# Attention inside a three-stage kernel: the ninth transpose block moves to the PSUM bank of the output rows

## The chip, the cores and the metric

The kernel runs on one core of one Trainium2 chip. The metric is the device time of one execution in microseconds (us). Three runs of the kernel before took 985.68, 984.39 and 983.36 us; the median is 984.39 us.

## The reference

The input is attention over 4 batches of 8 heads, 576 positions, head size 64. Its output goes through a mixture of 8 experts (2304 rows of 512, hidden size 1024) and then through a dense layer with hidden size 2048. Only the first stage is touched by the change:

```
scores = q @ k.T / 8
keep only scores >= rowmax - tau, the others become -1e9
attn = exp(scores - rowmax) / (sum + 1e-9)
x = attn @ v                                  # (4*576, 8*64)
expert of a row = argmax(x @ w_gate + modality_bias)
```

## The kernel before, in words

The attention phase handles the heads in 16 pairs. The 576 query rows of a pair are cut into 5 tiles: four of 128 queries (for both heads of the pair), and a fifth that holds the last 64 queries of both heads together. This gives 80 steps; step n has the tile number n % 5 (0 to 4). The fifth tile (n % 5 = 4) has half the score columns of the others. A batch is 20 steps.

A step passes through these pieces of work, each on its own engine and each some loop turns later than the one before. In loop turn c the engines issue, in this fixed order:

- TensorE: `scores(c)` (lines 419 to 426), `pv(c-4)` (the V products, lines 494, 497, 509), `rows_out(c-5)` (a product that turns the outputs back into rows and forms the gate logits, lines 526 and 532), `turn(c-2)` (transposes of the probabilities, lines 448 for most tiles, 471 to 477 for tile 1), and once in a batch, at its turn number 7, `ranks` (lines 537 and 538).
- VectorE: `copy_scores(c)` twice (line 705: scores out of PSUM, with the row minimum), `invert`, `probs(c-1)` twice (line 718: mask, multiply, sum), `normalise(c-5)` for tiles 1, 3 and 4 (lines 746 or 750 and 752: rows out of PSUM), then small pieces of the routing (`choose`, `place`, `fill_rows` and others) in the 15 to 18 turns of a batch after the first batch is done.
- ScalarE: `exps(c)` first half (line 583), `copy_out(c-4)` (line 606: V products out of PSUM), `exps(c)` second half, `evacuate(c-2)` (lines 592 to 599: first the rest block of the transposes, then the main part), and in 16 turns `lead_high` (line 613).
- GpSimd: `find_limit(c)` (line 339), `add_eps`, and weight splitting or scatters in some turns.

Each engine works through its list in order, and a wait at one piece holds all that is behind it on that engine. Scores have one set of banks, so `scores(c)` waits until VectorE has copied the scores of turn c-1. `turn(c-2)` waits until ScalarE has evacuated the turn before it.

The eight PSUM banks: 0 to 3 hold scores, 4 and 5 the main part of the transposes (`turn_bank`). A full tile has nine blocks to transpose and eight fit in banks 4 and 5; the ninth (`rest_bank`) lies in bank 6, columns 0 to 127. The output of the V products (`ot_bank`) lies in the same bank 6, columns 128 to 255. Bank 7 holds the ranks (columns 0 to 47), one moved column (48) and the rows of `rows_out` (`row_bank`, columns 224 to 511). Tile 4 has only eight blocks and does not use `rest_bank`. Because ScalarE reads the V products out of bank 6, the first transpose into bank 6 has a wait of its own, `other_bank()`: step n waits until `copy_out(n-2)` is done. For tiles 0, 2 and 3 this wait stands ahead of the first transpose of the step, for tile 1 ahead of the last one.

```
def other_bank():
    if n >= 2:
        pe.wait_ge(ot_out, min(n - 1, NS - 3))
```

Of the kernel before, what the change touches and what calls it, by code (L numbers as in the profile page):

```python
# [21 lines left out]
P = 128  # L22
B, H, S, D = 4, 8, 576, 64
# [70 lines left out]
def attention_phase(nc, t, io):  # L94
# [107 lines left out]

    ahead_in_p = bterm[:, 0:TT + 1]
    a_bank, b_bank = psum[:, 0:2, 0:HALF], psum[:, 2:4, 0:HALF]
    turn_bank, rest_bank = psum[:, 4:6, :], psum[:, 6, 0:P]
    FAR = S

    def by_half(n):
# [194 lines left out]
    def tensor(pe):  # L403
# [24 lines left out]
        def turn(n):  # L428
            w, full = n % 3, n % TT < QT
            if n == 0:  # L430
                pe.wait_ge(consts, ALL_CONSTS)
            pe.wait_ge(prob_done, units(n) + 1)
            if n >= 1:
                pe.wait_ge(main_out, n)
            if n >= 1:
                pe.wait_ge(rest_out, n)
            blocks = QT if not full else 2 * QT

            def other_bank():

                if n >= 2:
                    pe.wait_ge(ot_out, min(n - 1, NS - 3))

            if by_half(n):
                def half_block(place, h, b):
                    rows = slice(h * D, h * D + D)
                    key = b * P if b < QT else (S + REM + (b - QT) * P if b < 2 * QT else QT * P)
                    return pe.transpose(place, prob[rows, w, key:key + P], ident[rows, rows])  # L448

                if full:  # L450
                    other_bank()
                    half_block(rest_bank[:, D:2 * D], 1, 0).then_inc(far_turned, 1)
                else:
                    half_block(turn_bank[:, 1, 0:D], 1, 0)
                half_block(turn_bank[:, 0, 0:D], 0, 0)
                for b in range(1, blocks):
                    if b == QT:
                        pe.wait_ge(prob_done, units(n + 1))
                    at = b - full
                    half_block(turn_bank[:, 1, at * D:at * D + D], 1, b)  # L460
                    half_block(turn_bank[:, 0, b * D:b * D + D], 0, b)
                at = blocks - full
                half_block(turn_bank[:, 1, at * D:at * D + D], 1, 2 * QT)
                if full:
                    pe.wait_ge(far_turned, halved(n))
                    half_block(rest_bank[:, 0:D], 0, 2 * QT).then_inc(turned, 1)
                else:
                    half_block(turn_bank[:, 0, QT * D:QT * D + D], 0, 2 * QT).then_inc(turned, 1)
                return
            for j in range(QT):  # L470
                pe.transpose(turn_bank[:, 0, j * P:(j + 1) * P], prob[:, w, j * P:(j + 1) * P], ident[:])
            pe.wait_ge(prob_done, units(n + 1))
            for j in range(QT):
                pe.transpose(turn_bank[:, 1, j * P:(j + 1) * P],
                             prob[:, w, S + REM + j * P:S + REM + (j + 1) * P], ident[:])
            other_bank()
            pe.transpose(rest_bank, prob[:, w, QT * P:QT * P + P], ident[:]).then_inc(turned, 1)

        def pv(n):
            p, tt = divmod(n, TT)  # L480
            u, w = p % 2, n % 2
            if tt == 0:
                pe.wait_ge(v_in[u], 16 * (p // 2 + 1))
            pe.wait_ge(main_out, n + 1)
            pe.wait_ge(rest_out, n + 2 if n < NS - 3 else n + 1)
            if n == NS - 3:
                pe.wait_ge(copied, units(NS - 1))
            elif 1 <= n < NS - 1:
                pe.wait_ge(ot_out, n)
            ot = ot_bank(n)  # L490
            if tt < QT:
                for j in range(QT):
                    for h in range(2):
                        pe.matmul(ot[h * D:(h + 1) * D, :], vsb[:, u, (h * QT + j) * D:(h * QT + j + 1) * D],  # L494
                                  turned_block(n, h * QT + j), start=(j == 0), stop=False)
                for h in range(2):
                    last = pe.matmul(ot[h * D:(h + 1) * D, :], vsb[:, u, VBD + h * D:VBD + (h + 1) * D],
                                     turned_block(n, 2 * QT), start=False, stop=True)
                last.then_inc(pv_done, 1)
            else:  # L500
                for j in range(QT + 1):
                    for h in range(2):
                        if j < QT:
                            v = vsb[:, u, VTURN + j * D:VTURN + (j + 1) * D] if h else vsb[:, u, j * D:(j + 1) * D]
                            pr = pt[:, w, h * FAR + j * D:h * FAR + (j + 1) * D]
                        else:
                            v = vsb[:, u, VREST + h * D:VREST + (h + 1) * D]
                            pr = pt[:, w, h * FAR + QT * D:h * FAR + (QT + 1) * D]
                        last = pe.matmul(ot[h * D:(h + 1) * D, 0:REM], v, pr, start=(j == 0), stop=(j == QT))
                last.then_inc(pv_done, 1)  # L510

        def rows_out(n):

            p, tt = divmod(n, TT)
            if n == 0:
                pe.wait_ge(wx_done, 4 * HP)
            pe.wait_ge(ot_out, n + 1)
            if n >= 1:
                pe.wait_ge(x_done, norms(n))
            b, k = divmod(n + 4 - ROUTE - RANK, PER)  # L520
            if k == 0 and b >= 0:
                pe.wait_ge(ranks_read, b + 1)
            c = (tt % 2) * 2 * HW
            for h in range(2):
                rows = slice(h * D, h * D + D)
                last = pe.matmul(row_bank[rows, c:c + 2 * HW], otsb[:, n % 2, rows],
                                 wx[:, p % HP].rearrange("p h c -> p (h c)"), start=True, stop=True)
            if tt == QT:
                pe.wait_ge(summed, norms(n + 1))
                for h in range(2):  # L530
                    rows = slice(h * D, h * D + D)
                    last = pe.matmul(moved[rows], t["shift"][:, rows], rsum[:, p % 2, 2 * QT:TPP], start=True, stop=True)
            last.then_inc(rows_done, 1)
# [7 lines left out]
        for c in range(NS):  # L541
            scores(c)
            if c >= 4:
                pv(c - 4)
            if c >= 5:
                rows_out(c - 5)
            if c >= 2:
                turn(c - 2)
            b, k = divmod(c - ROUTE, PER)
            if b >= 0 and k == RANK:  # L550
                ranks(b)
        turn_x, up_half, down = early["pe"](pe)
        pv(NS - 4)
        pe.wait_ge(copied, units(NS - 1))
# [104 lines left out]
    def vector(dve):  # L659
# [74 lines left out]
        def normalise(n):  # L734
            p, tt = divmod(n, TT)
            b, i = divmod(p, HP)
            if tt % 2 == 0 and tt < QT:
                return
            if i == 0 and tt == 1 and b >= 2:
                dve.wait_ge(scattered, 16 * TT * (b - 1))  # L740
            dve.wait_ge(rows_done, n + 1)
            cols = slice(i * 2 * HW, (i + 1) * 2 * HW)
            if tt < QT:
                settled()
                r = rinv[:, 2 * tt - 2:2 * tt + 2].rearrange("p (t h) -> p t h", h=2).unsqueeze(3)
                dve.tensor_tensor(x[:, b % 2, tt - 1:tt + 1, cols].rearrange("p t (h c) -> p t h c", h=2),
                                  row_bank.rearrange("p (t h c) -> p t h c", t=2, h=2),
                                  r.to_broadcast([P, 2, 2, HW]), ALU.mult).then_inc(x_done, 1)
            else:
                step(dve.reciprocal(rinv[0:REM, TPP:TPP + 1], moved[0:REM]))  # L750
                r = rinv[0:REM, 2 * QT:2 * TT].unsqueeze(2)
                dve.tensor_tensor(x[0:REM, b % 2, QT, cols].rearrange("p (h c) -> p h c", h=2),
                                  row_bank[0:REM, 0:2 * HW].rearrange("p (h c) -> p h c", h=2),
                                  r.to_broadcast([REM, 2, HW]), ALU.mult).then_inc(x_done, 1)
# [31 lines left out]
        def place(b, k):  # L786
# [2 lines left out]
            settled()  # L789
            if k == 0:  # L790
                dve.wait_ge(rank_done, b + 1)
                ranks = rank_bank.rearrange("p (t e) -> p t e", e=E)
                note(dve.tensor_tensor(lg[:], ranks[:, 0:TT], base8[:].unsqueeze(1).to_broadcast(wide), ALU.add))
                settled()
# [929 lines left out]
```

## Time and profile before

| | us |
|---|---|
| median of three runs | 984.39 |
| the profiled execution | 985.06 |
| its span, first to last instruction | 983.4 |
| TensorE busy | 919.6 (94%) |
| VectorE busy | 676.5 (69%) |
| ScalarE busy | 513.5 (52%) |
| GpSimd busy | 478.1 (49%) |
| mean granted TensorE clock | 0.994 |

The attention phase takes roughly the first third of the span; the experts and the dense layer take the rest. The busy shares are means over all phases, so they do not say what limits the attention phase.

### The profile page before, as it was taken

How to read it: one execution, taken by the hardware profiler on the slowest of the kernel's cores; microseconds unless marked ns; L12 is line 12 of the kernel's file. 1: busy time of each engine (PE TensorE's matmuls, PEld its weight loads, DVE VectorE, ACT ScalarE, POOL GpSimd, SP SyncE). 2: the span in 40 equal slices, each digit the busy share in tenths (PEclk: the TensorE clock that was granted, in tenths of full speed). 3: DMA queues.
4: the chain of work that ended last, by engine and by line, in shares of the span. 5: the costliest groups of instructions: out<-in, count | busy, mean ns of one | idle time of the engine just before them, and what ended most of it. 6: DMA issues, size and time to landing. Idle time of an engine off the chain costs nothing.

```text
span 983.4 us, 19418 instructions
## 1 busy us (share of the span) xinstructions
PE 919.6 (94%) x6976; PEld 773.0 (79%) x6977; DVE 676.5 (69%) x1227; ACT 513.5 (52%) x987; POOL 478.1 (49%) x560
## 2 busy tenths in 40 slices
PE   6888898889889999999999997999999999999997
PEld 4676676667667878888887896888988899889995
DVE  6887888788875641111125399888888888888793
ACT  5666666777665242222235455555455545555452
POOL 4222225465432275300000077786777786777784
PEclk9999999999999999999999999999999999999999
DMA  3122128223212457211125300100100100000000
GB/s 125 50 75 73 50 56 323 80 74 110 69 35 68 168 175 244 77 45 45 47 76 198 116 1 0 34 33 1 32 33 1 32 33 1 15 18 1 33 1 33
DMA packets 21937, 65.97 MB, mean 67 GB/s; under 512 B 3552, under 2 KB 3552, under 8 KB 21600
## 3 DMA queue, kind: packets, MB, share of 16 engines
q1 hardware_dynamic: 14512, 39.90, 12.0%
q0 software_dynamic: 4896, 20.00, 6.1%
q10 hardware_dynamic: 2448, 5.01, 1.7%
q8 instruction: 49, 0.80, 0.3%
q14 instruction: 32, 0.26, 0.1%
HBM read 46.63 MB, written 18.27 MB: 66 GB/s over the span
## 4 chain that ended last, share of the span: by engine, by line
PE 59%; DVE 5%; issue 3%; ACT 1%; ACTq 0%; POOL 0%; DVEq 0%; POOLq 0%
PE psum L1419 6%; PE psum L1421 6%; PE psum L1420 6%; PE psum L1411 6%; PE psum L1409 6%; PE psum L1410 6%; PE psum L1082 3%; PE psum L1084 3%; PE psum L1083 3%; PE psum L1109 3%; PE psum L1111 3%; PE psum L1110 3%; DVE rr L1531 2%; PE psum L1093 2%; PE psum L1068 1%
## 5 line engine op out<-in xcount | busy, mean ns | idle before, releaser
L1531 DVE RECIPROCAL rr<-rr 128x384 f32<-128x384 f32 x96 | 244.1, 2543 | 10.0 <-ACT rr L1479 10.0
L583 ACT ACTIVATE prob<-ssb,smin 128x576 f32<-128x576 f32 x144 | 111.6, 776 | 72.2 <-DVE ssb L705 72.2
L1357 POOL TENSOR_TENSOR uu<-uu,ex 128x384 f32<-128x384 f32 x96 | 97.3, 1014 | 100.6 <-ACT uu L1473 100.6
L705 DVE TENSOR_SCALAR_CACHE_REDUCE ssb<-psum,tauk 128x576 f32<-128x576 f32 x144 | 112.5, 815 | 46.7 <-PE psum L422 46.2
L1409 PE MATMUL psum<-x2T_hi,w_in_hi 128*128 128x384 f32 x384 | 130.8, 341 | 4.3 <-DVE gg L1537 2.7
L339 POOL TENSOR_TENSOR limit<-smin,margin 128x2 f32<-128x2 f32 (+1 forms) x80 | 58.1, 726 | 152.2 <-DVE ssb L705 151.7
L1411 PE MATMUL psum<-x2T_hi,w_in_lo 128*128 128x384 f32 x384 | 129.3, 337 | 0.0
L1410 PE MATMUL psum<-x2T_lo,w_in_hi 128*128 128x384 f32 x384 | 128.7, 335 | 0.0
L1163 DVE TENSOR_TENSOR hT_lo<-psum,hT_hi 128x512 fp32r<-128x512 f32 x38 | 26.3, 691 | 140.8 <-ACT hT_hi L1140 140.8
L1419 PE MATMUL psum<-w_hi,g_hi 128*128 128x512 f32 x288 | 114.0, 396 | 0.1
L1421 PE MATMUL psum<-w_hi,g_lo 128*128 128x512 f32 x288 | 113.8, 395 | 0.0
L1420 PE MATMUL psum<-w_lo,g_hi 128*128 128x512 f32 x288 | 113.7, 395 | 0.0
L1479 ACT ACTIVATE rr<-uu 128x384 f32<-128x384 f32 x96 | 50.5, 526 | 118.6 <-POOL uu L1357 118.6
L1363 POOL TENSOR_TENSOR rr<-uu,rr 128x384 f32<-128x384 f32 x96 | 97.7, 1018 | 28.6 <-DVE rr L1531 28.4
L718 DVE SCALAR_TENSOR_TENSOR prob<-ssb,limit,prob 128x576 f32<-128x576 f32 x144 | 111.4, 807 | 0.1
L1368 POOL TENSOR_TENSOR g_lo<-gg,g_hi 128x384 fp32r<-128x384 f32 x96 | 101.6, 1058 | 1.5 <-ACT g_hi L1485 1.1
L1134 ACT ACTIVATE hid<-psum 128x512 f32<-128x512 f32 x38 | 22.7, 598 | 122.1 <-PE psum L1084 122.0
L448 PE MATMUL psum<-ident,prob 64*128 64x64 f32 x1024 | 45.7, 227 | 39.1 <-ACT otsb L606 39.1
L1470 ACT ACTIVATE ex<-ex 128x384 f32<-128x384 f32 x96 | 50.5, 526 | 59.7 <-DVE ex L1526 59.7
L448 PEld LDWEIGHTS psum<-ident,prob 64*128 64x128 f32 x1024 | 38.3, 138 | 51.5 <-issue 34.1
L1409 PEld LDWEIGHTS psum<-x2T_hi,w_in_hi 128*128 128x128 f32 x384 | 72.1, 188 | 8.3 <-DVE gg L1537 3.6
L494 PEld LDWEIGHTS psum<-pt,vsb 128*64 128x64 f32 x1024 | 56.1, 139 | 24.6 <-issue 23.8
(210 smaller groups left out, 2173.2 us busy)
## 6 DMA issues: line engine op xcount, KB each, us to landing
qk<-in_qk_dram SPq DMA_DIRECT2D x15, 640.0 KB, 3.9
vsb<-in_v_dram SPq DMA_DIRECT2D x16, 512.0 KB, 3.6
xrow<-xs ACTq DMA_DIRECT2D x17, 288.0 KB, 2.9
ys<-ysb SPq DMA_DIRECT2D x19, 257.0 KB, 3.1
stage<-in_w_in_dram POOLq DMA_DIRECT2D x16, 256.0 KB, 3.9
wa<-in_wa_dram SPq DMA_DIRECT2D x8, 512.0 KB, 7.1
wb<-in_wb_dram SPq DMA_DIRECT2D x8, 512.0 KB, 10.7
xs<-zrow SPq DMA_DIRECT2D x11, 288.0 KB, 3.0
```

The lines of the kernel that those rows point to most:

```text
L583: act.activation(prob[:, n % 3, cols], ssb[:, w, cols], ACT.Exp, bias=smin[:, w, h:h + 1], scale=-1.0).then_inc(exp_done, 1)
L705: dve.tensor_scalar(ssb[:, w, h * S:(h + 1) * S].rearrange("p (a q) -> p a q", a=2), banks(n)[h], factor, BIG, ALU.mult, ALU.min, accum_ou ...
L718: dve.scalar_tensor_tensor(out=prob[:, n % 3, cols], in0=ssb[:, w, cols], scalar=limit[:, w, h:h + 1], in1=prob[:, n % 3, cols], op0=ALU.i ...
L1363: pool.tensor_tensor(rr[:, n % 4], uu[:, n % 2], rr[:, n % 4], ALU.mult).then_inc(q_done, 1)
L1368: pool.tensor_tensor(g_lo[:, n % 4], gg[:, n % 2], g_hi[:, n % 4].bitcast(F32), ALU.subtract).then_inc(g_lo_done, 1)
L1409: pe.matmul(bank_of(n), w_in_hi[:, k, cols], xT_hi[w][:, k], start=(k == 0), stop=False)
L1410: pe.matmul(bank_of(n), w_in_hi[:, k, cols], xT_lo[w][:, k], start=False, stop=False)
L1411: last = pe.matmul(bank_of(n), w_in_lo[:, k, cols], xT_hi[w][:, k], start=False, stop=(k == KT - 1))
L1419: pe.matmul(out_bank[j], g_hi[:, n % 4, q], w_out_hi[half][:, fh], start=(f == 0), stop=False)
L1420: pe.matmul(out_bank[j], g_hi[:, n % 4, q], w_out_lo[half][:, fh], start=False, stop=False)
L1421: return pe.matmul(out_bank[j], g_lo[:, n % 4, q], w_out_hi[half][:, fh], start=False, stop=(f == FT2 - 1))
L1531: dve.reciprocal(rr[:, n % 4], rr[:, n % 4]).then_inc(r_done, 1)
```

## The change

The ninth block moves from bank 6 to bank 7, columns 64 to 191. Bank 6 is left to the V products, and `other_bank()` goes. Since bank 7 is read by VectorE (`normalise`, `place`) and written by `rows_out` and `ranks`, new waits on `rest_out` (ScalarE has copied the ninth block) are added: in `rows_out` on TensorE, and in `normalise` and `place` on VectorE. `pv` loses one step of its wait on `rest_out`. In the one turn of a batch that has `ranks`, these are issued before the transposes instead of after them.

```diff
-    turn_bank, rest_bank = psum[:, 4:6, :], psum[:, 6, 0:P]
+    turn_bank, rest_bank = psum[:, 4:6, :], psum[:, 7, D:D + P]
 # in turn(n), TensorE
-            def other_bank():
-
-                if n >= 2:
-                    pe.wait_ge(ot_out, min(n - 1, NS - 3))
-
                 if full:
-                    other_bank()
                     half_block(rest_bank[:, D:2 * D], 1, 0).then_inc(far_turned, 1)
...
-            other_bank()
             pe.transpose(rest_bank, prob[:, w, QT * P:QT * P + P], ident[:]).then_inc(turned, 1)
 # in pv(n), TensorE
-            pe.wait_ge(rest_out, n + 2 if n < NS - 3 else n + 1)
+            pe.wait_ge(rest_out, n + 1)
 # in rows_out(n), TensorE
             pe.wait_ge(ot_out, n + 1)
+            pe.wait_ge(rest_out, min(n + 3, NS))
 # the loop on TensorE
-            if c >= 2:
-                turn(c - 2)
             b, k = divmod(c - ROUTE, PER)
             if b >= 0 and k == RANK:
                 ranks(b)
+            if c >= 2:
+                turn(c - 2)
 # in normalise(n), VectorE
             dve.wait_ge(rows_done, n + 1)
+            if n + 3 < NS and (n + 3) % TT < QT:
+                dve.wait_ge(rest_out, n + 4)
 # in place(b, 0), VectorE
                 dve.wait_ge(rank_done, b + 1)
+                if b < B - 1:
+                    dve.wait_ge(rest_out, ROUTE + b * PER + RANK - 1)
```

The wait in `normalise(n)` applies to tiles 3 and 4 (for tile 1, step n+3 is a tile 4, which has no ninth block).

## Rows read from the trace of the kernel before

**Rows 1.** Who waited for whom, 21.48 to 303.68 us: total us, times, longest.

```profile
DVE ssb L705 <- PE psum L422: 45.2, 44, 2.2
PE psum L448 <- ACT otsb L606: 37.3, 42, 2.0
```

**Rows 2.** Attention in stretches: length, then busy us (instructions) of each engine, clock, DMA.

```profile
core 0: us, PE busy (x) PEld busy (x) DVE busy (x) ACT busy (x) POOL busy (x), PEclk, DMA share, GB/s
21.48:94.31 72.83, 64.15 (x934) 51.02 (x936) 60.37 (x178) 50.17 (x97) 17.45 (x32) 1.00 0.21 67
94.31:133.84 39.53, 34.28 (x472) 27.02 (x474) 33.26 (x107) 25.34 (x50) 8.72 (x16) 0.96 0.20 61
133.84:170.36 36.52, 32.08 (x468) 25.52 (x470) 30.50 (x94) 25.09 (x49) 16.71 (x23) 1.00 0.56 203
170.36:211.76 41.40, 34.58 (x472) 27.22 (x474) 35.11 (x106) 29.48 (x58) 20.35 (x24) 0.96 0.28 94
211.76:248.03 36.27, 32.08 (x468) 25.49 (x470) 29.71 (x86) 27.16 (x53) 20.16 (x26) 1.00 0.33 104
248.03:289.14 41.11, 34.32 (x472) 27.20 (x474) 34.62 (x107) 27.41 (x54) 15.15 (x21) 0.96 0.15 43
289.14:303.68 14.54, 13.06 (x189) 10.26 (x191) 12.45 (x38) 10.57 (x21) 8.55 (x11) 1.00 0.27 94
```

**Rows 3.** VectorE in order of time: start us, duration us, instruction, [idle before <-releaser].

```profile
43.40 0.82 DVE L705 TENSOR_SCALAR_CACHE_REDUCE ssb<-psum,tauk 128x576 f32<-128x576 f32 x1 [1.48 <-PE psum L422]
...
46.79 0.81 DVE L705 TENSOR_SCALAR_CACHE_REDUCE ssb<-psum,tauk 128x576 f32<-128x576 f32 x1
...
48.26 0.82 DVE L718 SCALAR_TENSOR_TENSOR prob<-ssb,limit,prob 128x576 f32<-128x576 f32 x1
...
50.57 0.82 DVE L705 TENSOR_SCALAR_CACHE_REDUCE ssb<-psum,tauk 128x576 f32<-128x576 f32 x1 [0.66 <-PE psum L422]
...
56.32 0.15 DVE L750 RECIPROCAL rinv<-psum 64x1 f32<-64x1 f32 x1
```

**Rows 4.** ScalarE in order of time, the same stretch.

```profile
47.64 0.78 ACT L583 ACTIVATE prob<-ssb,smin 128x576 f32<-128x576 f32 x1 [1.14 <-DVE ssb L705]
48.33 0.25 ACT L606 COPY otsb<-psum 128x128 f32<-128x128 f32 x1
...
49.69 1.02 ACT L596 COPY pt<-psum 128x1024 f32<-128x1024 f32 x1
...
56.78 0.27 ACT L595 COPY pt<-psum 128x128 f32<-128x128 f32 x1 [0.95 <-PE psum L448]
```

**Rows 5.** TensorE's weight loads in order of time, turns 11 to 15.

```profile
44.31 0.25 PEld L526 LDWEIGHTS psum<-wx,otsb 128*64 128x64 f32 x4
44.76 0.39 PEld L448 LDWEIGHTS psum<-ident,prob 64*128 64x128 f32 x10 [0.20 <-issue]
45.06 0.19 PEld L420 LDWEIGHTS psum<-qk 64*128 64x128 f32 x1
...
46.24 0.85 PEld L494 LDWEIGHTS psum<-pt,vsb 128*64 128x64 f32 x16 [0.38 <-issue]
...
47.28 0.25 PEld L526 LDWEIGHTS psum<-wx,otsb 128*64 128x64 f32 x4
48.69 0.67 PEld L448 LDWEIGHTS psum<-ident,prob 64*128 64x128 f32 x18 [1.16 <-issue]
49.24 0.19 PEld L420 LDWEIGHTS psum<-qk 64*128 64x128 f32 x1
...
50.45 0.66 PEld L509 LDWEIGHTS psum<-pt,vsb 128*64 128x64 f32 x20 [0.39 <-issue]
...
52.36 0.36 PEld L425 LDWEIGHTS psum<-qk 128*128 128x128 f32 x2
...
55.94 0.67 PEld L448 LDWEIGHTS psum<-ident,prob 64*128 64x128 f32 x18 [0.81 <-DVE prob L718]
56.49 0.19 PEld L420 LDWEIGHTS psum<-qk 64*128 64x128 f32 x1
```

## The prediction

> **What bounds the kernel now.** The table of waits comes first [rows 1]. Over 74 of the 80 attention turns VectorE stands 45.2 us, 44 times, at its first scores copy (line 705) for the last scores product, and TensorE stands 37.3 us, 42 times, at the transposes of line 448 for ScalarE's copy of the V products (line 606). The busy times by stretch come next [rows 2]: in each, TensorE and VectorE are both busy 80 to 90% and neither is full. So no engine is the bound. A ring through three of them is, and the time-ordered rows show it for turn 12 [rows 3 to 5]: VectorE starts the first scores copy at 46.79, ScalarE starts the exponential of it at 47.64 and the V product copy, which stands behind that, at 48.33 (0.25 long). TensorE begins the transposes at 48.69, the next scores at 49.24, and VectorE has them at 50.57. From copy to copy this is 3.78 us, though VectorE stood for 0.66 of it and TensorE for 1.16. The reader is to see that the transposes do not need the V product copy for their data: it is the shared bank alone.
>
> Turn 11 is the same without that wait. Its transposes are of a tile 4, which has no ninth block: they begin at 44.76, right behind the row product of 44.31, and VectorE goes from 43.40 to 46.79 in 3.39 us with no standing at the end [rows 3, 5].
>
> At 55.94 the row of the transposes names VectorE's probabilities as the releaser [rows 5]. I do not take that: the transposes of turn 14 need the probabilities of step 12, and VectorE makes those in turn 13, which was over before. The V product copy is the only other late input, so I count these with the 37.3 us.
>
> **Part 1: the wait for the V product copy goes.** What is late next on TensorE? Its own queue. I read its work in a turn as the distance between weight loads [rows 5]: scores 1.21 (49.24 to 50.45), V products 1.04 (46.24 to 47.28), rows 0.45 (44.31 to 44.76), transposes 0.55 (48.69 to 49.24). By the turn number c % 5:
> - 0: 1.21 + 1.04 + 0.45 + 0.55 = 3.25.
> - 1: 1.18 + 1.04 + 0.75 (44.31 to 45.06) = 2.97.
> - 2: 4.18 (45.06 to 49.24) less 0.96 of standing (48.69 - 47.28 - 0.45) = 3.22.
> - 3: 3.12 (49.24 to 52.36), where the wait stands only ahead of the last transpose and hides.
> - 4: 4.13 (52.36 to 56.49) less 0.61 (the 0.81 shown, less the 0.20 gap that also turn 11 has without a wait) = 3.52.
>
> Together 16.1 us for five turns. VectorE's own time is the DVE column: 60.37 for 20 turns is 15.1 for five in the plain stretches, and 33.26, 35.11 and 34.62 for ten (17 to 17.6 for five) where the routing runs [rows 2]. So plain turns become bound by TensorE, those with routing by VectorE.
>
> I check that nothing else holds a plain turn, with S the start of scores(c). VectorE's copy starts at S + 1.33 (49.24 to 50.57), both copies are done about 1.5 later (46.79 to 48.26) and, with 0.1 for the signal, scores(c+1) may start from S + 2.9; TensorE is free at S + 3.2. It is TensorE, by 0.3. ScalarE runs exponential, V copy, exponential, rest block, main copy from S + 2.2 to S + 4.9 (the main copy is 1.02 long [rows 4]); the next transposes come at S + 3.2 + 2.7 = S + 5.9, so the main copy is 1.0 early. In the 16 turns with a weight cast on ScalarE this cover shrinks to about 0.4, still enough. The qk and V loads are issued five or more turns ahead and stay hidden.
>
> Where VectorE is the bound, the turn with the tile-4 probabilities still leaves it short of work, since it has one probability pass less and TensorE needs its 3.25; I add 0.6 for every five turns.
>
> The sum over the stretches [rows 2], before and after: 72.83 becomes 4 x 16.1 + 0.2 = 64.6; 39.53 becomes 33.26 + 1.2 = 34.5; 36.52 becomes 32.4; 41.40 becomes 35.11 + 1.2 = 36.3; 36.27 becomes 32.2; 41.11 becomes 34.62 + 1.2 = 35.8; the last four turns, 14.54, become 12.9. That is 282.2 before and 248.7 after: 33.5 us. The ends of this term: not more than VectorE's standing, 45.2, and not less than 0 if something else holds the transposes where they are. I take 33.5, because turn 11 shows what a turn looks like without the wait.
>
> **Part 2: the new wait of normalise on VectorE.** It costs if ScalarE's rest-block copy ends after the second probability pass, and it would be paid on an engine that is nearly full. Turn 14 before: the rest block is copied 56.78 to 57.05, VectorE is at the reciprocal of normalise at 56.32 [rows 3, 4]. Unmoved transposes would cost 0.73 there, about 15 times: 11 us. With the transposes starting 0.61 earlier against the same scores, I get 0.1 to 0.2, in turns where VectorE has slack against TensorE: taken at 0.5 us in all, bounds 0 and 11. For tile 3 the probability passes end at S + 4.4 and the rest copy at S + 3.8: nothing. Queued behind the wait are the reciprocal, the row product's x, and the next scores copy; rows_out of the next turn waits for x, with some 0.7 us to spare.
>
> **Part 3: rows_out waits for the rest copy of the turn before, pv for one less.** That copy ended more than 1 us before rows_out is reached, and pv, ahead of it in the queue, had this same wait. Nothing, bounds 0 and 1 us.
>
> **Part 4: ranks ahead of the transposes; place waits for the rest block.** Three times. TensorE's work is the same; VectorE gets the ranks 0.5 us earlier and must wait for a rest block that comes 0.5 later. Nothing, bounds -1 and +1 us.
>
> The PSUM page of the Trainium skill ("PSUM bank collisions raise a hardware error") says that any two engines in one bank and the same partitions collide, two readers included, at whatever columns. By it none of the new waits could be left out, and Part 2's wait is the price of the move; the rows agree only in that the kernel before pays such a wait in bank 6.
>
> **Part 5: the clock.** Three stretches show a granted clock of 0.96, the others 1.00 [rows 2]: in each of the three some 3 us ran at the lower level, 1.2 GHz (0.04 x 40 us, twice). They are the ones with the long routing turns, where TensorE stands longest. At half clock 3 us of TensorE work is 1.5 late, so 4.5 us in all. My sum leaves these out altogether; with VectorE the bound part of the standing stays, so I give back a third, 1.5 us.
>
> TensorE: Matmul & The Clock Gate ("HAM oscillation", Trainium skill) says that waits between bursts of matmuls put the clock down again. The trace agrees, with 0.96 only where the standing is longest. By that rule alone, with the gaps shorter, all three drops would go, and the time would be 1.5 us under my forecast.
>
> **Sum.** The profiled execution took 985.06 (span 983.4 and 1.7 around it). 985.06 - 33.5 + 0.5 + 1.5 = 953.6; the median of the runs lies 0.7 under the profiled one, which gives 952.9, so 953.
>
> **Rivals.**
> - R1, gain partly lost to VectorE's new wait: the rest copy stands behind the second exponential, and transposes do not move as far forward as reckoned, so VectorE stands 0.4 to 0.7 us at most normalise calls of tiles 3 and 4 (30 of them), 12 to 20 us. For it: VectorE is the fuller engine in half of the turns. Against: before, tile 3's rest copy was already in time. 985 - 33.5 + 1.5 + 16 = 969.
> - R2, slower: the transposes are held by another input at the same time as before (the releaser of 55.94 is then right), and nothing is gained, while the wait in normalise costs 0.73 us about 15 times, plus 1 us for place. It decides from the point where the transposes start less than 0.7 us earlier and scores no earlier. Time: 996. Against: the 42 waits at line 448 name the V copy, and turn 11 runs on.
> - R3, the wait only changes its name: transposes free, but scores(c+1) then waits for VectorE's second copy so that nothing is gained: 984.5. Against: that ring is 2.9 us, 0.3 below TensorE's own work.
> - R4, the gain is nearly all of VectorE's standing: 45 us, 940. It needs TensorE's turn to be under 3.1 us.
>
> **Chances.** Forecast 0.70 (946 to 961), R1 0.12, R4 0.06, R2 0.07, R3 0.05. Range for eight in ten: 944 to 967. A measurement of this kernel tells 0.2%, 2 us, from no change: faster 0.89, same 0.04, slower 0.07.
>
> **What would show it.** In the profile after, TensorE's waits at line 448 for ScalarE line 606 are gone and VectorE's waits at line 705 fall from 45 to some 12 us. Plain groups of five turns take about 16.1 us. The first wait of rest_out in normalise shows as short gaps ahead of line 750; if they sum to 10 us or more, Part 2 is wrong. If line 448 waits for something new for over 0.5 us a turn, Part 1 is wrong. The experts and the dense layer should take the same time as before.

## The result, and the profile after

The changed kernel takes 951.34 us (median of four runs, 950.58 to 953.41) against 984.31 us (the three runs of the kernel before and a fourth, 984.22). The ratio is 0.9667, 95% interval 0.9647 to 0.9688: faster by 33 us. The forecast was 953 us with a range of 944 to 967.

The span fell from 983.4 to 948.9 us, 34.5 us. Line numbers moved: the scores copy is now line 699 (was 705), the transposes 443 (448), ScalarE's V product copy 600 (606), normalise 742 and 746 (746 and 750). The table of waits of the kernel after, over the same turns as [rows 1] (20.19 to 270.78 us):

```profile
DVE ssb L699 <- PE psum L422: 10.2, 17, 0.9
...
DVE x L742 <- DMA xs<-x,slots: 2.3, 1, 2.3
PE psum L520 <- DVE x L742: 2.2, 2, 1.9
```

VectorE's standing for scores fell from 45.2 to 10.2 us, and no row of transposes waiting for the V product copy is left. Two of the new rows stand below, both mainly from one place; they come up again under the loads. The same stretches as [rows 2], with the same columns:

```profile
20.19:84.05 63.86, 63.73 (x934) 50.31 (x930) 60.20 (x178) 48.96 (x96) 17.68 (x33) 1.00 0.24 76
84.05:118.22 34.17, 33.57 (x480) 26.34 (x482) 32.84 (x107) 24.70 (x50) 8.72 (x16) 1.00 0.22 71
118.22:149.81 31.59, 31.59 (x464) 24.93 (x460) 30.38 (x95) 24.56 (x48) 15.64 (x23) 1.00 0.54 205
149.81:189.05 39.24, 35.53 (x484) 27.69 (x486) 35.15 (x106) 28.83 (x59) 19.46 (x24) 0.96 0.36 123
189.05:221.43 32.38, 31.82 (x460) 24.75 (x458) 30.51 (x87) 26.51 (x53) 20.10 (x26) 1.00 0.37 116
221.43:256.66 35.23, 33.65 (x480) 26.51 (x482) 34.26 (x107) 26.74 (x54) 16.18 (x21) 1.00 0.16 51
256.66:270.78 14.12, 13.07 (x185) 10.17 (x181) 12.49 (x40) 10.47 (x21) 8.14 (x11) 1.00 0.27 96
```

TensorE's busy column now nearly fills the plain stretches (63.73 of 63.86), and VectorE's column has hardly moved. The stretches of turns 25 to 34, 45 to 54 and 65 to 74 are those where the routing runs; the others are plain. Side by side, in us:

| turns | before | forecast | after |
|---|---|---|---|
| 5 to 24 | 72.83 | 64.6 | 63.86 |
| 25 to 34 | 39.53 | 34.5 | 34.17 |
| 35 to 44 | 36.52 | 32.4 | 31.59 |
| 45 to 54 | 41.40 | 36.3 | 39.24 |
| 55 to 64 | 36.27 | 32.2 | 32.38 |
| 65 to 74 | 41.11 | 35.8 | 35.23 |
| 75 to 78 | 14.54 | 12.9 | 14.12 |
| sum | 282.2 | 248.7 | 250.6 |

These turns give 31.6 of the 34.5 us. The start gives 1.3 (turn 5 at 20.19 instead of 21.48); all behind turn 79 gives 1.6 (983.4 - 303.68 = 679.7, and 948.9 - 270.78 = 678.1). The start is not steady: over the three profiles of the changed kernel turn 5 came at 20.1 to 21.3, so 1 us there is no finding. The 1.6 us behind turn 79 were not looked into; the prediction had taken that part as unchanged.

Turn 12 after, to be read against [rows 3 to 5], all three engines from their own views in order of time:

```profile
42.56 0.81 DVE L699 TENSOR_SCALAR_CACHE_REDUCE ssb<-psum,tauk 128x576 f32<-128x576 f32 x1
...
43.41 0.78 ACT L577 ACTIVATE prob<-ssb,smin 128x576 f32<-128x576 f32 x1 [1.14 <-DVE ssb L699]
...
43.50 0.64 PEld L443 LDWEIGHTS psum<-ident,prob 64*128 64x128 f32 x18 [0.20 <-issue]
...
44.09 0.25 ACT L600 COPY otsb<-psum 128x128 f32<-128x128 f32 x1
...
44.16 0.18 PEld L419 LDWEIGHTS psum<-qk 64*128 64x128 f32 x1
...
45.70 0.82 DVE L699 TENSOR_SCALAR_CACHE_REDUCE ssb<-psum,tauk 128x576 f32<-128x576 f32 x1
```

The transposes start at 43.50, before the V product copy (44.09) and not 0.36 after it. The turn takes 3.14 us instead of 3.78. Counted between the first weight loads of the scores, turns 15, 11, 12, 13 and 14 take 3.21, 2.97, 3.33, 3.15 and 3.28 us, where Part 1 had 3.25, 2.97, 3.22, 3.12 and 3.52: its terms hold, and not only their sum. The new wait of normalise, at turn 14:

```profile
50.85 0.27 ACT L589 COPY pt<-psum 128x128 f32<-128x128 f32 x1
...
51.45 0.16 DVE L746 RECIPROCAL rinv<-psum 64x1 f32<-64x1 f32 x1
```

The rest block is copied by 51.12, a third of a microsecond before VectorE gets there. In the whole trace after, line 746 never stands for ScalarE.

### The profile page after: what moved, and what is told of

Same layout as the page of the kernel before. It is cut to its first block, busy times and chain, and to the rows that moved or that the text cites. A ratio compares the mean times of both kernels' runs of the same rounds, so it can differ in the third digit from the quotient of the medians.

```text
span 948.9 us, 19389 instructions
## 1 busy us (share of the span) xinstructions
PE 919.1 (97%) x6976; PEld 771.2 (81%) x6977; DVE 675.5 (71%) x1227; ACT 509.0 (54%) x987; POOL 476.6 (50%) x560
## 4 chain that ended last, share of the span: by engine, by line
PE 61%; DVE 4%; issue 4%; ACT 1%; ACTq 1%; POOL 0%; POOLq 0%; DVEq 0%
PE psum L1417 6%; PE psum L1419 6%; PE psum L1418 6%; PE psum L1409 6%; PE psum L1407 6%; PE psum L1408 6%; PE psum L1080 3%; PE psum L1082 3%; PE psum L1081 3%; PE psum L1107 3%; PE psum L1109 3%; PE psum L1108 3%; DVE rr L1529 2%; PE psum L1091 2%; PE psum L1066 1%
## 5 line engine op out<-in xcount | busy, mean ns | idle before, releaser
L1524 DVE TENSOR_SCALAR ex<-psum 128x384 f32<-128x384 f32 x96 | 52.8, 550 | 31.4 <-PE psum L1409 31.4
L1408 PEld LDWEIGHTS psum<-x2T_lo,w_in_hi 128*128 128x128 f32 x384 | 72.3, 188 | 3.1
```

The source lines that it names most:

```text
L1408: pe.matmul(bank_of(n), w_in_hi[:, k, cols], xT_lo[w][:, k], start=False, stop=False)
```

## The experiments

Each kernel ran beside the kernel before, and ratios are to that. The times under one "Measured" come from one chip; where kernels from different chips are compared, only their ratios to the kernel before count, since the changed kernel's own time differed by 1.2 us from one chip to another.

**The wait put back.**

```diff
                 if full:
+                    if n >= 2:
+                        pe.wait_ge(ot_out, min(n - 1, NS - 3))
                     half_block(rest_bank[:, D:2 * D], 1, 0)...
...
+            if n >= 2:
+                pe.wait_ge(ot_out, min(n - 1, NS - 3))
             pe.transpose(rest_bank, prob[:, w, QT * P:QT * P + P], ident[:])...
```

> The changed kernel with the wait for the V product copy put back ahead of the first transpose of tiles 0, 2, 3 and the last of tile 1; the bank, the new waits and the order of the ranks stay as changed. Theory (the whole gain is the removed wait, and the new wait in normalise is free only because the transposes moved forward): the gain of 33 us goes and normalise stands up to 0.73 us in some 15 turns, 984 to 995 us. Rival A (the new waits cost nothing in either place): 982 to 985. Rival B (the gain comes from the eased wait of pv or from the ranks): stays at 951 to 956.

Measured: 982.08 us, ratio 0.997 (0.9957 to 0.9983), 2 us under the range of the theory. Against the ratio of the changed kernel, 0.9667, the removed wait is worth about 30 us, and what else changed about 3. Rival B falls for the 30. Its table of waits (20 to 285 us; here the scores copy is line 703 and the V product copy 604):

```profile
PE psum L443 <- ACT otsb L604: 35.7, 42, 2.0
DVE ssb L703 <- PE psum L422: 29.0, 34, 1.6
...
DVE rinv L750 <- ACT pt L593: 9.9, 13, 0.9
```

And one of those 13, in turn 14:

```profile
57.11 0.16 DVE L750 RECIPROCAL rinv<-psum 64x1 f32<-64x1 f32 x1 [0.75 <-ACT pt L593]
```

VectorE stands in the new wait just as reckoned (0.75, where 0.73 was forecast). Over the same turns as [rows 1] (21.45 to 300.87 us in this kernel) the three rows read 37.1, 31.1 and 10.6 us. But the time doesn't grow. The kernel to hold it against is the kernel before with only the ranks moved (the last experiment below): it has the same time and none of the new waits, and its VectorE stands 43.3 us for scores over these turns. So 10.6 us of new standing came, and 12.2 us of the old went: VectorE would have stood for the next scores anyway. Here a wait on an engine that stands later in the same turn was free up to the length of that standing. Rival A was right on the time for this reason, not because the wait was empty.

**The wait put back for tile 1 alone** (only the second of the two edits above).

> The changed kernel with the wait put back only ahead of the last transpose of tile 1. Theory (it hides there, since eight other transposes and the V product copy run at the same time): 951 to 954 us. Rival (with the turns shorter the copy is late there as well, about 0.5 us in 16 turns): 959.

Measured: 952.69 us, 0.9669 (0.965 to 0.9689), not to be told from the changed kernel. Its profile shows 16.1 to 16.7 us for plain groups of five turns, where the changed kernel has 15.7 to 16.4, and TensorE's weight loads stand 7.4 us in 15 turns for the V product copy. Without turns 45 to 49, whose length moves for another reason (see the loads), turns 5 to 74 are 2.3 us longer, so most of the 7.4 is given back in the same group. It mostly hides.

**More work on one engine.**

```diff
-            for h in range(2):
+            for h in (0, 1, 0, 1):
                 rows = slice(h * D, h * D + D)
                 last = pe.matmul(row_bank[rows, c:c + 2 * HW], ...
```

> The changed kernel with the row product of every step issued twice (TensorE work alone, about 0.23 us in 80 turns, 18 us in all, the same result). Theory (TensorE bounds the turns without routing, about 50 of 80, and VectorE the others): plus 10 to 14 us, 961 to 965, with the plain groups of five turns 1.1 us longer and the routing groups by less than 0.6. Rival A (TensorE bounds everywhere): plus 18, 969. Rival B (VectorE bounds everywhere): plus 0 to 3, 951 to 954.

```diff
             if 5 <= c:
+            settled()
+            note(dve.memset(trow[:, 0]..., 0.0))
                 invert(c - 5)
```

(The memset stands ahead of the `if`, in every turn.)

> The changed kernel with a memset of 240 numbers on one partition added to VectorE's work in every turn (some 0.15 to 0.25 us). Theory (VectorE bounds the 30 turns with routing and has 0.2 us a turn to spare in the plain ones): plus 4 to 8 us, 955 to 959. Rival A (TensorE bounds everywhere): plus 0 to 1, 952. Rival B (VectorE bounds everywhere): plus 12 to 20, 963 to 971.

Measured: 960.39 us (0.9751, 0.9735 to 0.9767) and 961.95 us (0.9762, 0.9745 to 0.978). The group lengths, from the first scores copy of each fifth turn, tell more than the totals:

| group of turns | changed | TensorE more | VectorE more |
|---|---|---|---|
| 10 to 14, plain | 16.14 | 17.00 | 16.60 |
| 20 to 24, plain | 15.94 | 17.00 | 16.27 |
| 30 to 34, routing | 17.04 | 17.40 | 17.76 |
| 50 to 54, routing | 18.56 | 18.60 | 19.47 |
| 70 to 74, routing | 17.04 | 17.09 | 17.75 |

The three profiles of the changed kernel agree in these five groups within 0.02 us, but for 50 to 54 (18.55 to 18.89).

The added matmuls (about 1.1 us in five turns) show nearly in full in plain groups and hardly in routing groups: TensorE bounds the first and VectorE the second, as forecast. The memset measured 258 ns, 1.3 us in five turns; 0.7 to 0.9 of it shows in these routing groups and 0.3 to 0.5 in the plain ones, so plain turns have less room on VectorE than I had reckoned. The groups left out of the table say the same less sharply: the other plain ones grow by 0.4 to 1.2 us with more on TensorE and by 0.3 to 0.8 with more on VectorE, 65 to 69 by 0.24 and 0.80. In 25 to 29, counted with the routing, neither shows (0.23 and 0.13), so which engine bounds these five turns stays open. TensorE's total came out 0.6 us under its range and VectorE's 3 us above. In VectorE's profile the turns 5 to 79 take 6.4 to 8.0 us more than in the three profiles of the changed kernel, which is the forecast; the rest is mostly a start 1.5 to 2.7 us later (turn 5 at 22.8), and the start is unsteady.

**The loads and the scatters.** In the kernel after, turn 46 took 6.14 us against 3.74 before, and here are the instructions behind the two new rows of the table of waits:

```profile
158.44 0.46 DVE L742 TENSOR_TENSOR x<-psum,rinv 128x288 f32<-128x288 f32 x1 [2.31 <-DMA xs<-x,slots]
...
159.05 0.47 PE L520 MATMUL psum<-wx,otsb 128*64 128x144 f32 x4 [1.85 <-DVE x L742]
```

VectorE may not write the third batch's rows over the first's until GpSimd's five scatters of the first batch have landed. Behind the second of them GpSimd issues 4 MB of the lead expert's weights, so three scatters come behind the loads. The second load and the last scatter:

```profile
139.16 0.58 POOL L368 DMA_DIRECT2D wb<-in_wb_dram  x1
...
146.19 1.34 POOL L361 DMA_INDIRECT xs<-x,slots  x1 [0.15 <-issue]
```

The second load took 15.7 us from issue to landing, to 154.9, and the last scatter, issued at 146.2, released VectorE only at 158.4. In the kernel before the last scatter was issued at 165.8 and VectorE came there at 177.2, 11.4 us later, and did not stand. Now it came after 9.9 us and stood until 12.2. In the other two profiles of the changed kernel this stand is 3.5 and 3.6 us. Two moves of the loads:

```diff
-            if c == LOAD_AT:
+            if c == LOAD_AT - 2:
```

> The changed kernel with the two loads of the lead expert's weights (4 MB, GpSimd's queue) issued two turns earlier, ahead of all five scatters of the first batch. Theory (in turn 46 VectorE stood 2.3 us for those scatters, because they are queued with the loads, and TensorE stood behind it): the stand and the low clock after it go, 3 to 5 us less, 946 to 948. Rival (the scatters behind both loads land later still): VectorE stands 2 to 6 us longer, 953 to 957.

```diff
-LOAD_AT = ROUTE + RANK + 8
+LOAD_AT = ROUTE + RANK + 12
```

> The changed kernel with the loads issued four turns later, behind the scatters of the first batch, and the casts that use them moved with them. Theory: the scatters land in time, turn 46 takes about 3.2 us instead of 6.1, 946 to 948. Rival (the casts now meet the routing turns of the third batch, or the weights are late): 950 to 955.

> The changed kernel itself, to be compared with the next three on the same chip: 951 us, 950 to 953.

Early: 956.15 us (0.9698, 0.9684 to 0.9713) against 951.22 (0.9655, 0.9641 to 0.9669) for the changed kernel on that chip. The stand in turn 46 does go (3.74 us, as before the change), but the time is the rival's, by a mechanism that neither names, in turn 41:

```profile
146.22 1.09 POOL L361 DMA_INDIRECT xs<-x,slots  x1 [10.91 <-DMA xs<-zrow]
147.65 0.82 DVE L712 SCALAR_TENSOR_TENSOR prob<-ssb,limit,prob 128x576 f32<-128x576 f32 x1 [7.58 <-issue]
```

The first scatter has to follow three clearing writes (288 KB each) from another queue, and those now land beside the 4 MB: up to 11.8 us from issue, where the kernel after has 2.7 to 3.1. GpSimd waits 10.9 us for them and works out its next limits only behind the scatter, at 147.35. VectorE stands 7.6 us; its row names no releaser, and the limits are the input that came just then. Late: 949.65 us (0.9634, 0.9621 to 0.9648), above the 946 to 948 of the theory and with intervals overlapping. In its profile the stand is gone and turns 45 to 49 took 16.76 us instead of 20.7 to 22.9 (turn 46 itself 3.74, not 3.2). Both kernels were measured once more, with a variant on top of the edit above:

```diff
-SPLIT_AT = [c for c in range(LOAD_AT + 6, NS) ...
+SPLIT_AT = [c for c in range(LOAD_AT + 4, NS) ...
```

> The changed kernel once more, as the measure for the next two: 951 us, 950 to 952.

> The kernel with the weight loads behind the scatters again, the same code. Its profile had turns 45 to 49 in 16.8 us instead of 20.7 to 21.8 and turns 70 to 74 about 1.1 longer. Theory (the gain is real and the first profile only had a slow start of 2.7 us): 947 to 949 us. Rival (no gain over the changed kernel): 951.

> The loads four turns later, and the weight casts and splits two turns after that move instead of four, so that they end in turn 69 and stay out of turns 70 and 71. Theory (the first weights land 2.7 turns after the issue, in time): 1 us less than the run before, 946 to 949. Rival (the casts wait for the weights and hold ScalarE): 950 to 953.

Measured: changed kernel 952.43 us (0.9665, 0.9649 to 0.9681; 950 to 952 was expected), loads late 948.27 (0.9627, 0.961 to 0.9644), splits sooner 946.98 (0.9612, 0.9596 to 0.9629). The last is 5.4 us under the changed kernel with intervals apart, and is the fastest version here; its 1.3 us against loads late lie within the intervals, though turns 70 to 74 show them. Its turns 45 to 49 took 16.77 us and turns 70 to 74 took 17.04, where loads late had 18.12. The last variant's turns 45 to 54 took 35.32 us, where 36.3 was forecast and the changed kernel had 39.24, and no longer fall to the lower clock (0.96 in the changed kernel, above):

```profile
149.00:189.00 40.00, 38.43 (x562) 30.46 (x560) 38.96 (x120) 31.36 (x63) 19.97 (x28) 1.00 0.54 197
```

**The order of the ranks.**

```diff
+            if c >= 2:
+                turn(c - 2)
             if b >= 0 and k == RANK:
+                pe.wait_ge(rest_out, c - 1)
                 ranks(b)
-            if c >= 2:
-                turn(c - 2)
```

> The changed kernel with the ranks behind the transposes again, which needs a wait of TensorE for the copy of the ninth block ahead of them, three times. Theory (Part 4: the order is worth nothing, but the wait now stands on TensorE 0.4 us and the ranks come about 1 us later to VectorE, which is the bound in these turns): plus 1 to 3 us, 952 to 954. Rival (hidden): 951.

And the other way about, the kernel before with only the ranks moved ahead:

> The kernel before with only the ranks moved ahead of the transposes, nothing else. The kernel with the wait put back was 3 us under the kernel before though its transposes stood as long; in its profile the three groups of turns with ranks were 0.5 to 1.5 us shorter. Theory (the ranks ahead use time in which TensorE stands for the V product copy anyway, and take 0.5 us out of the path three times, with the low clock that follows): minus 2 to 4 us, 981 to 983. Rival (worth nothing, as Part 4 had it; the 3 us came from the eased wait of pv): 984 to 985.

Ranks behind, in the changed kernel: 957.62 us (0.9731, 0.9705 to 0.9758) against 951.22, so 6.4 us and not 1 to 3. The wait costs more than its copy is long:

```profile
111.58 0.78 ACT L578 ACTIVATE prob<-ssb,smin 128x576 f32<-128x576 f32 x1
112.25 0.25 ACT L590 COPY pt<-psum 128x128 f32<-128x128 f32 x1
...
112.56 0.30 PEld L531 LDWEIGHTS psum<-oh,ltri 128*128 128x128 f32 x2 [1.57 <-ACT pt L590]
```

The copy stands behind the second exponential, so TensorE stands 1.57 us (4.7 us over the three times), and with it the ranks and the next scores. Right after, the clock drops (0.50 from 114 to 117 us; 0.92 in 101 to 122 us, where the changed kernel has 1.00). This kernel has one wait more than the changed one, so it does not price the order alone. Ranks ahead alone: 982.06 us, 0.9965 (0.9953 to 0.9978), 3.4 us under the kernel before and the same as the kernel with the wait put back. So the 3 us that were left there are the ranks' order. In the kernel before, the ranks took TensorE 0.58 us (123.57 to 124.15) between the transposes and the next scores, right behind a stand of 1.41 us for the V product copy; moved ahead, they run in place of a part of that stand, which shrinks to 0.84 us, and turn 32 takes 3.77 us instead of 5.07. VectorE's standing for the ranks goes as well; this row of the kernel before is not in the table of the other:

```profile
DVE lg L793 <- PE psum L538: 1.0, 3, 0.3
```

Groups 30 to 34, 50 to 54 and 70 to 74 took 18.97, 20.37 and 19.63 instead of 20.57, 21.40 and 20.52; and the granted clock of about these three stretches, first before, then with the ranks ahead:

```profile
113.27:133.84 20.57, 18.24 (x239) 14.25 (x241) 16.75 (x55) 12.79 (x26) 4.36 (x8) 0.92 0.19 58
190.36:211.76 21.40, 18.21 (x239) 14.45 (x241) 17.91 (x54) 15.06 (x30) 11.60 (x13) 0.94 0.18 56
268.00:289.00 21.00, 18.56 (x241) 14.44 (x237) 16.70 (x54) 13.07 (x26) 4.35 (x8) 0.92 0.09 27
```

```profile
113.00:133.00 20.00, 17.64 (x249) 13.86 (x246) 16.82 (x56) 13.62 (x27) 4.38 (x9) 1.00 0.19 61
190.00:211.00 21.00, 17.41 (x251) 13.74 (x247) 18.64 (x57) 15.75 (x31) 11.84 (x13) 1.00 0.18 58
268.00:289.00 21.00, 18.43 (x267) 14.85 (x266) 17.95 (x59) 14.16 (x28) 5.07 (x9) 0.98 0.09 26
```

How much of the 3.4 us is the clock and how much the shorter queue of TensorE the runs do not separate; VectorE's standing for the ranks, three times 0.3, is at most 1 us of it. The kernel with the wait put back, which has the ranks ahead too, shows 1.00 in all three stretches.

## Why the prediction was right

- **The bound** (a ring through three engines, closed by the shared bank): shown. Putting one wait back brings 30 of the 33 us back.
- **Part 1**, 33.5 us: the turns gave 31.6, of which the wait alone is about 30. The sum counts the turns after from the engines' own work, so it took the gain of the ranks' order (Part 4) with it unnoticed. Its working holds as well as its total: the plain stretches came within 0.9 us of the forecast (the last four turns 1.2 over), with TensorE the bound, and the routing stretches within 0.6 us but for turns 45 to 54, 2.9 us over. That the bound of the routing turns is VectorE is shown for 30 to 34, 50 to 54, 65 to 69 and 70 to 74. The releaser named at 55.94 [rows 5] was rightly distrusted: the stand went with the V product wait.
- **Part 2**, 0.5 us: nothing was measured in the changed kernel. The room is small, though: with the doubled row product the same wait stood 3.2 us in 9 turns. Its price when the transposes stay, 11 us, was right as standing (10.6 us) and wrong as time. That is the step of R2 that failed: it added VectorE's new stand to the turn, without asking whether VectorE stands later in that turn. As the kernel with the wait put back shows, transposes that stay where they were give 982 (985 without the gain of the ranks' order), not 996.
- **Part 3**, nothing: agrees, since ranks-first alone and the wait put back, which differ in the bank and the new waits, have the same ratio (0.9965 and 0.997). It was not tested by itself.
- **Part 4**, nothing: wrong, 3.4 us gained in the kernel before, where Part 4 allowed 1; in the changed kernel the order was not priced by itself. The step that failed is "TensorE's work is the same": it is, but the ranks behind the transposes came after a stand of TensorE and ahead of scores that VectorE waited for, and TensorE ran on at the lower clock.
- **Part 5**, 1.5 us given back: two of the three stretches at 0.96 went to 1.00. The third stayed at 0.96, behind the stand of turn 46 (VectorE 2.3 us, TensorE 1.9); with the scatters in time it too is at 1.00. That a stand of TensorE comes before each drop was right; what takes it away was not the removed wait alone. With the V product wait still in place (36.9 us) the ranks' order, which Part 4 had at nothing, brought about these three stretches to 1.00, 1.00 and 0.98. Without that wait, but with the ranks behind and waiting for the rest copy, the first was at 0.92. The rule of the Trainium skill's page TensorE: Matmul & The Clock Gate ("HAM oscillation"), that waits between bursts bring the clock down, agrees with this: the lower clock came behind stands of TensorE of 1.41 us in turn 32 before, 1.57 us in the kernel with the ranks behind, and 1.85 us in turn 46 after.
- **Not in the prediction**: the scatters. It checked the loads of q, k and V for cover in the shorter turns, and not the other transfers that VectorE waits for. This cost about 5 us against the best order of the loads, and 2.9 us against the forecast for turns 45 to 54. In the span this is made up for by the 2.0 us of Parts 2 and 5, which did not come, by the start (1.3 us) and by the 1.6 us behind turn 79. That 951.3 lies within 2 us of 953 is partly luck, because these misses cancel.
- Of the rivals, R2 is answered above. R1's partial stand and R3's ring did not come: VectorE's standing for scores is 10.2 us (forecast 12).

## What to carry to other kernels

When a wait is removed from a ring, compute each engine's own work per turn, and take the longest as the new turn; then list every transfer that was hidden by the old, longer turns and check each against the new length. Here a new wait cost only what it added beyond the standing that already followed it in the same turn, which was nothing. Two things that only shared a PSUM bank were as tightly bound as two that share data (30 us for one wait), so look which of a bank's tenants is read late.

## What the runs showed that I had not expected

The 4 MB load stretched smaller transfers beside it far beyond their own length: clearing writes that land in 2.7 to 3.1 us took up to 11.8 and held the first scatter 10.9 us in one kernel. In another a scatter issued at 146.2 released its reader at 158.4; it is in the loads' own queue, and whether it waited there for its turn or for the bandwidth no run separates. And 0.6 us of work, moved from behind to ahead of a stand, was worth 3.4 us over three uses, with the granted clock of the three stretches going from 0.92, 0.94 and 0.92 to 1.00, 1.00 and 0.98.
